# Moving side work between engines in a recurrence-plus-dense kernel: weight remainders to VectorE, weighing to ScalarE, eight full-height turns, and a new order of steps

## The chip, the cores and the metric

One Trainium2 chip, one core. The time is the device time of one execution in microseconds (us); less is better. Engines are named as the profile does: PE is TensorE, DVE is VectorE, ACT is ScalarE, POOL is GpSimd, SP is SyncE.

## The reference

Three layers over x of shape 4 x 768 x 384 (batch, sequence, model), all in fp32. The first is a recurrence for 4 batches and 8 heads of 48 features:

```
for t in range(768):
    y[t]  = r[t] @ (state + outer(u * k[t], v[t]))
    state = w[t][:, None] * state + outer(k[t], v[t])
# token and channel mixing
u2 = x + (relu(x.T @ w_tok1) @ w_tok2).T        # 768 -> 256 -> 768
x  = u2 + relu(u2 @ w_ch1) @ w_ch2              # 384 -> 1536 -> 384
# gated convolution, 5 taps along the sequence
out = (sigmoid(conv(x, conv_w)) * (x @ w_val)) @ w_out
```

## The kernel before

**The recurrence** is worked in super-units of 256 time steps of one batch: s = 0 to 11, three for each batch. Keys k and queries r of two heads lie on 112 partitions (48, 16 of zeros, 48), 1024 columns each. Inside chunks of 64 steps the decays are joined level by level: L1, L2, L4, L8, L16, L32. At level m TensorE multiplies 64 small products (L), VectorE multiplies half of r and k by decays (`carry`, 112x1024), joins the decays of the level four times as long (`join_decays`, a short product) and takes the products into the matrix A (`into_a`, a predicated copy). `carry(m)` of s waits for TensorE's L(m) of s, and TensorE's L(2m) waits for `carry(m)`. Before them stand F (the first level's operands: a copy of odd columns by ScalarE, and even columns times u, called weighing, by GpSimd) and W (the first decays and `carry(1)`, by VectorE). Behind them: T turns k so that time lies on partitions (TensorE, then a ScalarE copy out of PSUM into `kt_sides`), D makes the state products of the chunks (TensorE, ScalarE copies them to `ds`, GpSimd then steps through the states, `states(s)`), A and B give the outputs, and Z splits the result in a high and a low part (ScalarE, then VectorE).

**The dense layers** work on fp32r with each operand split into a high and a low part: three products for one. P and G1 are the first token product, U the second, C1 and C2 the channel products (6 groups for each tile of 256 tokens, 18 matmuls for each group), X, tap, gate, V, M, S, O the gated convolution.

**Weights** come in 20 chunks (w:0 to w:19) through two landing buffers that `gate` and `xf` lend. For each chunk ScalarE writes the high part, and another engine subtracts it to give the low part: VectorE for even chunks, GpSimd for odd ones. The chunk after next may land only when that is done (`w_lo`).

**Order.** Each engine runs its own queue in order. All queues are cut from one list of words: PROLOGUE (batch 0's recurrence, three super-units interleaved, and the first 11 weight chunks), TRIP three times (dense layers of one batch interleaved with the recurrence of the next; n in `L8:n` is the super-unit, 3 being the next batch's first, and `L8:0` the one that the prologue or the trip before began), and TAIL (dense layers of the last batch). A word that an engine has no part in costs it nothing. PSUM for the recurrence is three pairs of banks, in dense stretches two, filled in turn; a stage waits until what it overwrites has been taken out (`emptied`).

Of the kernel before, what the change touches and what calls it, by code (L numbers as in the profile page):

```python
# [5 lines left out]
F32 = mybir.dt.float32  # L6
# [42 lines left out]
def slot(par, p):  # L49
# [5 lines left out]


PROLOGUE = """
    F:0 W:0 L2:0 L1:0 F:1 W:1 L4:0 w:0 L2:1 L8:0 L4:1 F:2 L1:1 w:1 W:2 L16:0 L8:1 L2:2 L1:2 w:2 w:3 L4:2 L16:1
    L32:0 L8:2 w:4 L32:1 T:0 L16:2 D:0 w:5 L32:2 T:1 w:6 D:1 A:0 T:2 B:0 A:1 Z:0 F:3 w:7 w:8 B:1 D:2 Z:1 P:0
    L1:3 A:2 w:9 W:3 L2:3 w:10 B:2 Z:2 P:1 L4:3 P:2 G1.0.0 G1.0.1  # L60
"""
TRIP = """
    L8:0 w:11 U.0.0 w:12 L16:0 w:13 C1.0.0 L32:0 w:14 C1.0.1 T:0 w:15 w:16 C2.0.0 D:0 F:1 C1.0.2 W:1 C2.0.1
    C1.0.3 w:17 C2.0.2 A:0 L1:1 B:0 Z:0 C2.0.3 C1.0.4 L2:1 C1.0.5 L4:1 C2.0.4 w:18 w:19 C2.0.5 X.0.0 L8:1 U.1.0
    L16:1 C1.1.0 L32:1 C2.1.0 tap.0.0 tap.0.1 T:1 C1.1.1 tap.0.2 D:1 C1.1.2 gate.0.0 tap.0.3 V.0.0 A:1 M.0.0 B:1
    C2.1.1 Z:1 tap.0.4 gate.0.1 F:2 S.0.0 C2.1.2 M.0.1 W:2 S.0.1 C1.1.3 C1.1.4 L2:2 C2.1.3 L4:2 O.0.0 L8:2
    C1.1.5 L16:2 L1:2 C2.1.4 L32:2 C2.1.5 X.1.0 U.2.0 T:2 tap.1.0 C1.2.0 D:2 tap.1.1 tap.1.2 C1.2.1 gate.1.0
    tap.1.3 F:3 tap.1.4 C2.2.0 C1.2.2 A:2 V.1.0 W:3 gate.1.1 M.1.0 B:2 C2.2.1 M.1.1 Z:2 C1.2.3 C2.2.2 S.1.0
    S.1.1 O.1.0 L2:3 L1:3 C2.2.3 C1.2.4 C1.2.5 C2.2.4 C2.2.5 X.2.0 tap.2.0 tap.2.1 G1.0.0 tap.2.2 G1.0.1 V.2.0
    tap.2.3 gate.2.0 M.2.0 tap.2.4 gate.2.1 S.2.0 M.2.1 S.2.1 L4:3 O.2.0  # L70
"""
TAIL = """
    U.0.0 C1.0.0 C1.0.1 C2.0.0 C1.0.2 C2.0.1 C1.0.3 C2.0.2 C1.0.4 C2.0.3 C1.0.5 C2.0.4 C2.0.5 X.0.0 U.1.0
# [3 lines left out]
    C2.2.2 O.1.0 C1.2.4 C2.2.3 C1.2.5 C2.2.4 C2.2.5 X.2.0 tap.2.0 N.2.0 V.2.0 tap.2.1 tap.2.2 gate.2.0 tap.2.3  # L77
    M.2.0 tap.2.4 gate.2.1 S.2.0 M.2.1 S.2.1 N.2.1 O.2.0
"""
PAIR_STAGES = tuple(f"L{m}" for m in LEVELS) + ("T", "D", "A")  # L80


# [63 lines left out]
def landing(s):  # L146

    return {0: 2, 1: 0, 2: 3, 3: 1}.get(s, s % 2)
# [58 lines left out]
def build(nc, rk, v, w, u, mask_d, ident_d, tok1_d, tok2_d, ch1_d, ch2_d, val_d, conv_d, outw_d, y_out):  # L207
    ctx = ExitStack()
    with ctx:
# [130 lines left out]
        def emptied(s, name):  # L340

            if name == "T":
                return kt_sb, s + 1
            if name == "D":
                return ds_sb, s + 1
            if name == "A":
                return xl_done, s + 1
            return into_done[landing(s)], INTO[(s, name)] + copies(s, name)
# [62 lines left out]

        @block.gpsimd
        def _(pool):
            def split_weight(n):
                if n % 2 == 1:
                    name, c0, cols, _ = chunks[n]
                    pool.wait_ge(w_hi, n + 1)
                    nc.gpsimd.tensor_tensor(wt[name][:, LO, c0:c0 + cols], stage[1][:, 0:cols],
                                            wt[name][:, HI, c0:c0 + cols].bitcast(F32), ALU.subtract)\
                        .then_inc(w_lo[1], 1)  # L420

            def weigh(s):

                pool.wait_ge(rk_in[landing(s)], 16 * landings(s))
                need(pool, lev_done[1], 4 * tenant(s))
                plain, first = rk_sides[landing(s)][0:RD, 0:1], first_rk[home(s)][0:RD, 0:1]
                steps = [[PH * CH + 1, 2], [QS * CH, PAIRS], [2, SU // 2]]
                scale = bass.AP(ut.tensor, ut.offset, [[ut.ap[0][0], RD], [0, 2], [1, PAIRS], [0, SU // 2]])
                nc.gpsimd.tensor_tensor(bass.AP(first.tensor, first.offset, [list(first.ap[0])] + steps),
                                        bass.AP(plain.tensor, plain.offset, [list(plain.ap[0])] + steps),  # L430
                                        scale, ALU.mult).then_inc(weighed, 1)

            def states(s):

                first = QS * (s % SUPERS)
                need(pool, y_done, 4 * (s - 1))
                pool.wait_ge(decay_done[CH], s + 1)
                pool.wait_ge(ds_sb, s + 1)
                decay = decays(s, CH).rearrange("p (a q) -> p a q", q=QS)
                for q in range(chunks_of(s)):  # L440
                    now, new = st[0:RD, (first + q) % SLOTS], st[0:RD, (first + q + 1) % SLOTS]
                    if first + q == 0:
                        nc.gpsimd.tensor_copy(new, ds[0:RD, q]).then_inc(st_done, 1)
                    else:
                        pool.wait_ge(st_done, states_until(s, q))
                        nc.gpsimd.tensor_tensor(new, now, decay[:, :, q].unsqueeze(2).to_broadcast([RD, PAIRS, D]),  # L446
                                                ALU.mult).then_inc(st_decayed, 1)
                        pool.wait_ge(st_decayed, states_until(s, q) - s // SUPERS)
                        nc.gpsimd.tensor_tensor(new, new, ds[0:RD, q], ALU.add).then_inc(st_done, 1)  # L449

            pool.wait_ge(u_in, 16)
            for kind, n, name in PROGRAM:
                if kind == "weight":
                    split_weight(n)
                elif kind == "att" and name == "F":
                    weigh(n)
                elif kind == "att" and name == "D":
                    states(n)

        @block.scalar  # L460
        def _(act):
# [10 lines left out]
            def first_operands(s):  # L472
# [5 lines left out]
                copy(bass.AP(first.tensor, first.offset, [list(first.ap[0])] + steps),  # L478
                     bass.AP(plain.tensor, plain.offset, [list(plain.ap[0])] + steps)).then_inc(plain_done, 1)

            def att(s, name):
                if name == "F":
                    first_operands(s)
                elif s < SUPERS and name in BY_SCALAR:
                    bank, m = bank_of(s, name), int(name[1:])
                    act.wait_ge(lev_done[m], 4 * (s + 1))
# [7 lines left out]
                                .then_inc(into_done[landing(s)], 1)  # L494
                elif name == "T":
                    bank = bank_of(s, name)
                    act.wait_ge(kt_done, 4 * (s + 1))
                    copy(kt_sides[landing(s)].rearrange("p (w h) d -> p w (h d)", w=2),
                         ps[:, bank:bank + 2, 0:PH // 2 * D]).then_inc(kt_sb, 1)
                elif name == "D":  # L500
                    bank = bank_of(s, name)
                    n = chunks_of(s)
                    act.wait_ge(ds_done, 4 * (s + 1))
                    need(act, st_done, states_until(s, 0))
                    copy(ds[0:RD, 0:n, :, :].rearrange("p q (w a) d -> p w q (a d)", w=2),
                         ps[0:RD, bank:bank + 2, 0:n * 2 * D].rearrange("p w (q e) -> p w q e", q=n))\
                        .then_inc(ds_sb, 1)
                elif name == "Z":
                    bank = bank_of(s, "A")
                    b, i = divmod(s, SUPERS)  # L510
                    act.wait_ge(y_done, 4 * (s + 1))
                    if b:
                        act.wait_ge(mm_done, ring_filled(RING_USE[(b - 1, "U", i, 1)]))
                    copy(xs[:, HI, 2 * i:2 * i + 2, :], ps[:, bank:bank + 2, 0:DM]).then_inc(xh_done, 1)
# [67 lines left out]
        def _(dve):  # L582
# [2 lines left out]

            def split_weight(n):

                if n % 2 == 0:
                    name, c0, cols, _ = chunks[n]
                    dve.wait_ge(w_hi, n + 1)  # L590
                    nc.vector.tensor_tensor(wt[name][:, LO, c0:c0 + cols], stage[0][:, 0:cols],
                                            wt[name][:, HI, c0:c0 + cols].bitcast(F32), ALU.subtract)\
                        .then_inc(w_lo[0], 1)

            def join_decays(s, m):

# [9 lines left out]
            def carry(s, m):  # L606
# [10 lines left out]
                else:  # L617
                    dve.wait_ge(lev_done[m], 4 * (s + 1))
                    dve.wait_ge(decay_done[m], s + 1)
                    if m == 2:  # L620
                        dve.wait_ge(weighed, s + 1)
                mul(both, both, decay).then_inc(next_done[m], 1)

            def into_a(s, name):
# [139 lines left out]
        def _(pe):  # L764
# [28 lines left out]

            def turn_back(s, bank):

                for at0, (p2, q) in enumerate((p2, q) for p2 in range(2) for q in range(QS)):
                    for two in range(2):
                        ph = (2 * two + p2) * QS + q
                        for par in range(2):
                            rows, turn = slice(par * CH, par * CH + D), slot(par, 2 * two)  # L800
                            ins = mm(ps[turn * CH:(turn + 1) * CH, bank + two, at0 * D:(at0 + 1) * D],
                                     k_sides[landing(s)][rows, ph * CH:(ph + 1) * CH], ident[rows, rows], True)
                            if at0 == PH // 2 - 1:
                                ins.then_inc(kt_done, 1)

            def state_products(s, bank):

# [36 lines left out]
            def att(s, name):  # L844
# [3 lines left out]
                        pe.wait_ge(*emptied(*before))  # L848
                if name == "L1":
                    pe.wait_ge(plain_done, s + 1)  # L850
                    pe.wait_ge(weighed, s + 1)
                    scores(s, bank, CH, first_k[home(s)],
                           lambda rows, ph: first_r[home(s)][rows, ph * CH:(ph + 1) * CH], lev_done[1])
                elif name[0] == "L":
# [7 lines left out]
                    pe.wait_ge(next_done[CH // 2], s + 1)  # L862
                    turn_back(s, bank)
                elif name == "D":
                    pe.wait_ge(kt_sb, s + 1)
                    pe.wait_ge(v_in[s % 2], 16 * (s // 2 + 1))
                    state_products(s, bank)
                elif name == "A":
# [196 lines left out]
```

## Time and profile before

| | |
|---|---|
| median of 3 runs | 653.58 us (650.83 to 656.93) |
| the profiled execution | 653.66 us, span 651.9 us |
| busy: PE, PEld, DVE | 605.5, 583.3, 410.1 us |
| busy: ACT, POOL | 185.2, 97.2 us |
| mean granted clock of TensorE | 0.992 |
| chain that ended last | PE 80%, DVE 11%, issue 4%, ACT 2%, POOL 1% |

PE is time in matmuls, PEld in loading their stationary operand, which runs beside PE. The chain is followed back from the last instruction through whatever released each step; "issue" is time for which the profile shows no cause.

### The profile page before, as it was taken

The numbers are of one execution on the slowest core, as the hardware profiler recorded it, in microseconds if no ns is written. First come the engines' busy times: TensorE is split into PE (matmuls) and PEld (weight loads), VectorE is DVE, ScalarE is ACT, GpSimd is POOL, SyncE is SP. The second block draws the span as 40 slices with busy tenths as digits, with TensorE's granted clock in tenths as the row PEclk, the third lists the DMA queues.
The fourth block names the chain that finished last, engine by engine and source line by source line (L and its number), as shares of the span: only waits on it lengthen the run. The fifth ranks groups of instructions, "written<-read, shape, count | busy, mean of one in ns | idle before, by whom it ended". The sixth has DMA issues, their size and how long they took to land.

```text
span 651.9 us, 24065 instructions
## 1 busy us (share of the span) xinstructions
PE 605.5 (93%) x11150; PEld 583.3 (89%) x11150; DVE 410.1 (63%) x618; ACT 185.2 (28%) x323; POOL 97.2 (15%) x110
## 2 busy tenths in 40 slices
PE   3578688999999999999999999999999999999997
PEld 3477587999999999999999999998999989999997
DVE  6996567486678476486678476485676262452616
ACT  2135414224224132213223132213223132221312
POOL 2314812503003000404003000404002000000000
PEclk9999978999999999999999999999999999999999
DMA  9911643410301300300401300300000000000000
GB/s 248 256 29 53 176 132 99 128 34 4 112 27 39 98 1 28 88 25 4 111 28 44 93 1 27 98 17 3 3 27 2 25 7 19 2 1 25 1 25 25
DMA packets 13332, 35.27 MB, mean 54 GB/s; under 512 B 1584, under 2 KB 7984, under 8 KB 11888
## 3 DMA queue, kind: packets, MB, share of 16 engines
q1 hardware_dynamic: 9776, 29.01, 15.9%
q10 hardware_dynamic: 3456, 4.72, 2.0%
q8 instruction: 88, 1.44, 0.9%
q14 instruction: 12, 0.10, 0.1%
HBM read 29.01 MB, written 4.72 MB: 52 GB/s over the span
## 4 chain that ended last, share of the span: by engine, by line
PE 80%; DVE 11%; issue 4%; ACT 2%; DMA 1%; DVEq 1%; POOL 1%; SPq 0%; ACTq 0%; POOLq 0%
PE ps L766 80%; DVE rk L584 2%; DVE wp L584 2%; DVE at L644 1%; DMA w<-in_w_dram 1%; DVE gate L733 1%; DVE rk_next L584 1%; DVEq L708 1%; DVE us L692 1%; ACT x2s L463 1%; DVE x2s L720 1%; DVE xf L709 1%; DVE xf L713 1%; DVE gate L584 0%; DVE x_sum L673 0%
## 5 line engine op out<-in xcount | busy, mean ns | idle before, releaser
L766 PE MATMUL ps<-us,ch 128*128 128x256 f32 x1296 | 167.8, 284 | 2.3 <-DVE us L692 1.7
L766 PE MATMUL ps<-hid,ch 128*128 128x256 f32 x1296 | 165.9, 283 | 0.0
L766 PEld LDWEIGHTS ps<-us,ch 128*128 128x128 f32 x1296 | 158.1, 189 | 5.3 <-DVE us L692 2.9
L766 PEld LDWEIGHTS ps<-hid,ch 128*128 128x128 f32 x1296 | 157.1, 188 | 1.6
L677 DVE SCALAR_TENSOR_TENSOR hid<-ps,hid 128x512 fp32r<-128x512 f32 x72 | 49.7, 691 | 126.9 <-ACT hid L533 126.7
L533 ACT ACTIVATE hid<-ps 128x512 fp32r<-128x512 f32 x72 | 43.0, 598 | 163.0 <-PE ps L766 163.0
L733 DVE SCALAR_TENSOR_TENSOR gate<-xf,cw,gate 128x256 f32<-128x256 f32 x144 | 72.4, 548 | 3.7 <-ACT gate L549 2.7
L766 PE MATMUL ps<-rk 48*64 48x32 f32 (+1 forms) x2240 | 48.4, 244 | 24.8 <-DVE rk L584 19.4
L766 PEld LDWEIGHTS ps<-rk 48*64 48x64 f32 (+1 forms) x2240 | 44.6, 162 | 29.4 <-issue 26.1
L446 POOL TENSOR_TENSOR st<-st,wp 112x192 f32<-112x192 f32 x40 | 23.6, 590 | 194.3 <-ACT ds L463 191.8
L584 DVE TENSOR_TENSOR rk<-rk,wp 112x1024 f32<-112x1024 f32 x35 | 42.9, 1229 | 14.1 <-PE ps L766 14.1
L584 DVE TENSOR_TENSOR rk_next<-rk_next,wp 112x1024 f32<-112x1024 f32 x25 | 33.8, 1351 | 16.9 <-PE ps L766 16.9
L766 PE MATMUL ps<-outw,x2s 128*128 128x384 f32 x216 | 40.3, 339 | 2.0 <-ACT x2s L463 1.8
L766 PE MATMUL ps<-x2s,val 128*128 128x256 f32 x324 | 41.4, 284 | 0.0
L766 PEld LDWEIGHTS ps<-x2s,val 128*128 128x128 f32 x324 | 39.9, 191 | 0.4 <-DVE hid L677 0.2
L766 PEld LDWEIGHTS ps<-outw,x2s 128*128 128x128 f32 x216 | 36.7, 188 | 3.1 <-DVE gate L584 2.2
L644 DVE COPY_PREDICATED at<-masks,ps 128x512 f32<-128x512 uint8 (+1 forms) x36 | 33.7, 936 | 6.8 <-PE ps L766 5.8
L766 PEld LDWEIGHTS ps<-rk_next 48*64 48x64 f32 (+1 forms) x1600 | 24.4, 131 | 9.8 <-issue 7.9
L766 PE MATMUL ps<-rk_next 48*64 48x32 f32 (+1 forms) x1600 | 27.2, 217 | 5.5 <-DVE rk_next L584 5.3
L766 PE MATMUL ps<-tok,h 128*128 128x256 f32 x216 | 31.5, 290 | 0.3 <-DVE h L677 0.2
L644 DVE COPY_PREDICATED at_next<-masks,ps 128x512 f32<-128x512 uint8 (+1 forms) x30 | 27.3, 911 | 4.3 <-PE ps L766 4.0
L449 POOL TENSOR_TENSOR st<-st,ds 112x192 f32<-112x192 f32 x40 | 28.3, 707 | 3.1
(84 smaller groups left out, 630.1 us busy)
## 6 DMA issues: line engine op xcount, KB each, us to landing
rk<-in_rk_dram SPq DMA_DIRECT2D x7, 896.0 KB, 7.2
w<-in_w_dram SPq DMA_DIRECT2D x12, 448.0 KB, 4.2
vs<-in_v_dram SPq DMA_DIRECT2D x12, 384.0 KB, 7.1
out_dram<-gate ACTq DMA_DIRECT2D x24, 192.0 KB, 1.9
rk_next<-in_rk_dram SPq DMA_DIRECT2D x5, 896.0 KB, 6.6
gate<-in_moe_w_ch_dram SPq DMA_DIRECT2D x6, 384.0 KB, 3.3
xf<-in_moe_w_ch_dram SPq DMA_DIRECT2D x6, 384.0 KB, 3.4
gate<-in_moe_w_tok_dram SPq DMA_DIRECT2D x2, 384.0 KB, 9.7
```

Of the source, the lines that this page charges most:

```text
L446: nc.gpsimd.tensor_tensor(new, now, decay[:, :, q].unsqueeze(2).to_broadcast([RD, PAIRS, D]), ALU.mult).then_inc(st_decayed, 1)
L449: nc.gpsimd.tensor_tensor(new, new, ds[0:RD, q], ALU.add).then_inc(st_done, 1)
L463: return nc.scalar.activation(out, in_, ACT.Copy)
L533: nc.scalar.activation(hid[:, HI, g % 2, :], ps[:, RING + use % 2, :], ACT.Relu)\
L584: return nc.vector.tensor_tensor(out, a, b_, ALU.mult)
L644: nc.vector.copy_predicated(out, may.unsqueeze(1).to_broadcast(list(out.shape)), src)\
L677: return nc.vector.scalar_tensor_tensor(out, bank, 0.0, hi.bitcast(F32), ALU.max, ALU.subtract)
L692: nc.vector.tensor_tensor(us[:, LO, dts, :], bank, us[:, HI, dts, :].bitcast(F32), ALU.subtract).then_inc(ring_free[use % 2], 1)
L708: dve.drain()
L709: nc.vector.tensor_tensor(xf[:, :, HALO:], us[:, HI, :, :].bitcast(F32), us[:, LO, :, :].bitcast(F32), ALU.add)
L733: nc.vector.scalar_tensor_tensor(gate3[:, dt, :], xf[:, dt, k:k + TT], cw[:, dt, k:k + 1], gate3[:, dt, :], ALU.mult, ALU.add).then_inc(ta ...
L766: return nc.tensor.matmul(out, lhsT, rhs, start=start, stop=stop, skip_group_check=True, **kw)
```

## The change

Four edits:

- GpSimd makes no low parts of weights any more; VectorE makes all twenty, in its own order.
- Weighing (F) moves from one GpSimd instruction (112x1024) to four ScalarE instructions (112x256 each), behind ScalarE's own copy in F. `weighed` counts to 4 for each super-unit.
- T: 64 small matmuls against a 48x48 identity become eight full-height passes (112 rows, 128 columns of k, identity of 112 columns, transpose mode). ScalarE's single copy of 128x768 out of PSUM becomes four copies of 64x384, which put each quarter to its rows; `kt_sb` counts to 4.
- PROLOGUE and TRIP are in a new order: in the prologue L1:1, L16:1, L32:0, L1:3 and B:2 come earlier and L1:2 and L2:3 later; in the trip C2.0.2 moves behind Z:0, C1.0.0 before w:13, C1.0.4 and C1.0.5 behind one level each, tap.2.3 before G1.0.1. TAIL is unchanged.

```
-    F:0 W:0 L2:0 L1:0 F:1 W:1 L4:0 w:0 L2:1 L8:0 L4:1 F:2 L1:1 w:1 W:2 L16:0 L8:1 L2:2 L1:2 w:2 w:3 L4:2 L16:1
-    L32:0 L8:2 w:4 L32:1 T:0 L16:2 D:0 w:5 L32:2 T:1 w:6 D:1 A:0 T:2 B:0 A:1 Z:0 F:3 w:7 w:8 B:1 D:2 Z:1 P:0
-    L1:3 A:2 w:9 W:3 L2:3 w:10 B:2 Z:2 P:1 L4:3 P:2 G1.0.0 G1.0.1
+    F:0 W:0 L2:0 L1:0 F:1 W:1 L4:0 w:0 F:2 L1:1 L2:1 L8:0 L4:1 w:1 W:2 L16:0 L8:1 L2:2 L16:1 w:2 L32:0 w:3 L4:2
+    L1:2 L8:2 w:4 L32:1 T:0 L16:2 D:0 w:5 L32:2 T:1 w:6 D:1 A:0 T:2 B:0 A:1 w:7 Z:0 F:3 B:1 w:8 D:2 L1:3 Z:1 P:0
+    A:2 w:9 W:3 B:2 Z:2 L2:3 w:10 P:1 L4:3 P:2 G1.0.0 G1.0.1
-    L8:0 w:11 U.0.0 w:12 L16:0 w:13 C1.0.0 L32:0 w:14 C1.0.1 T:0 w:15 w:16 C2.0.0 D:0 F:1 C1.0.2 W:1 C2.0.1
-    C1.0.3 w:17 C2.0.2 A:0 L1:1 B:0 Z:0 C2.0.3 C1.0.4 L2:1 C1.0.5 L4:1 C2.0.4 w:18 w:19 C2.0.5 X.0.0 L8:1 U.1.0
+    L8:0 w:11 U.0.0 w:12 L16:0 C1.0.0 w:13 L32:0 w:14 C1.0.1 T:0 w:15 w:16 C2.0.0 D:0 F:1 C1.0.2 W:1 C2.0.1
+    C1.0.3 w:17 A:0 L1:1 B:0 Z:0 C2.0.2 C2.0.3 L2:1 C1.0.4 L4:1 C1.0.5 C2.0.4 w:18 w:19 C2.0.5 X.0.0 L8:1 U.1.0
-    S.1.1 O.1.0 L2:3 L1:3 C2.2.3 C1.2.4 C1.2.5 C2.2.4 C2.2.5 X.2.0 tap.2.0 tap.2.1 G1.0.0 tap.2.2 G1.0.1 V.2.0
-    tap.2.3 gate.2.0 M.2.0 tap.2.4 gate.2.1 S.2.0 M.2.1 S.2.1 L4:3 O.2.0
+    S.1.1 O.1.0 L2:3 L1:3 C2.2.3 C1.2.4 C1.2.5 C2.2.4 C2.2.5 X.2.0 tap.2.0 tap.2.1 G1.0.0 tap.2.2 tap.2.3 G1.0.1
+    V.2.0 gate.2.0 M.2.0 tap.2.4 gate.2.1 S.2.0 M.2.1 S.2.1 L4:3 O.2.0
...
+TURNS = ((0, 0), (1, 1), (0, 1), (1, 0))
...
-                return kt_sb, s + 1
+                return kt_sb, len(TURNS) * (s + 1)
...
-            def split_weight(n):
-                if n % 2 == 1:
-                    name, c0, cols, _ = chunks[n]
-                    pool.wait_ge(w_hi, n + 1)
-                    nc.gpsimd.tensor_tensor(wt[name][:, LO, c0:c0 + cols], stage[1][:, 0:cols],
-                                            wt[name][:, HI, c0:c0 + cols].bitcast(F32), ALU.subtract)\
-                        .then_inc(w_lo[1], 1)
...
-                nc.gpsimd.tensor_tensor(bass.AP(first.tensor, first.offset, [list(first.ap[0])] + steps),
-                                        bass.AP(plain.tensor, plain.offset, [list(plain.ap[0])] + steps),
-                                        scale, ALU.mult).then_inc(weighed, 1)
...
-                if kind == "weight":
-                    split_weight(n)
-                elif kind == "att" and name == "F":
-                    weigh(n)
-                elif kind == "att" and name == "D":
+                if kind == "att" and name == "D":
...
+            def weigh(s):
+
+
+                for p in range(PAIRS):
+                    at, steps = p * QS * CH, [[PH * CH + 1, 2], [2, SU // 2]]
+                    plain, first = rk_sides[landing(s)][0:RD, at:at + 1], first_rk[home(s)][0:RD, at:at + 1]
+                    nc.scalar.activation(bass.AP(first.tensor, first.offset, [list(first.ap[0])] + steps),
+                                         bass.AP(plain.tensor, plain.offset, [list(plain.ap[0])] + steps),
+                                         ACT.Copy, scale=ut[0:RD, p:p + 1]).then_inc(weighed, 1)
...
                     first_operands(s)
+                    if s == 0:
+                        act.wait_ge(u_in, 16)
+                    weigh(s)
...
-                    act.wait_ge(kt_done, 4 * (s + 1))
-                    copy(kt_sides[landing(s)].rearrange("p (w h) d -> p w (h d)", w=2),
-                         ps[:, bank:bank + 2, 0:PH // 2 * D]).then_inc(kt_sb, 1)
+                    act.wait_ge(kt_done, s + 1)
+                    for row, half in TURNS:
+
+                        to = kt_sides[landing(s)].rearrange("p (w n half) d -> p w n half d", w=2, half=2)
+                        turned = ps[half * CH:(half + 1) * CH, bank, slot(row, 0) * CH:slot(row, 0) * CH + 1]
+                        other = ps[half * CH:(half + 1) * CH, bank + 1, slot(row, 2) * CH:slot(row, 2) * CH + 1]
+                        copy(to[row * CH:(row + 1) * CH, :, :, half, :],
+                             bass.AP(turned.tensor, turned.offset,
+                                     [list(turned.ap[0]), [other.offset - turned.offset, 2], [RD, PH // 4], [1, D]]))\
+                            .then_inc(kt_sb, 1)
...
-                if n % 2 == 0:
-                    name, c0, cols, _ = chunks[n]
-                    dve.wait_ge(w_hi, n + 1)
-                    nc.vector.tensor_tensor(wt[name][:, LO, c0:c0 + cols], stage[0][:, 0:cols],
-                                            wt[name][:, HI, c0:c0 + cols].bitcast(F32), ALU.subtract)\
-                        .then_inc(w_lo[0], 1)
+                name, c0, cols, _ = chunks[n]
+                dve.wait_ge(w_hi, n + 1)
+                nc.vector.tensor_tensor(wt[name][:, LO, c0:c0 + cols], stage[n % 2][:, 0:cols],
+                                        wt[name][:, HI, c0:c0 + cols].bitcast(F32), ALU.subtract)\
+                    .then_inc(w_lo[n % 2], 1)
...
-                        dve.wait_ge(weighed, s + 1)
+                        dve.wait_ge(weighed, PAIRS * (s + 1))
...
-                            ins = mm(ps[turn * CH:(turn + 1) * CH, bank + two, at0 * D:(at0 + 1) * D],
-                                     k_sides[landing(s)][rows, ph * CH:(ph + 1) * CH], ident[rows, rows], True)
-                            if at0 == PH // 2 - 1:
-                                ins.then_inc(kt_done, 1)
+
+                for two in range(2):
+                    for n in range(PH // 4):
+                        first = (two * PH // 4 + n) * 2 * CH
+                        ins = mm(ps[:, bank + two, n * RD:(n + 1) * RD],
+                                 k_sides[landing(s)][0:RD, first:first + 2 * CH], ident[0:RD, 0:RD],
+                                 n == 0, is_transpose=True)
+                ins.then_inc(kt_done, 1)
...
-                    pe.wait_ge(weighed, s + 1)
+                    pe.wait_ge(weighed, PAIRS * (s + 1))
...
-                    pe.wait_ge(kt_sb, s + 1)
+                    pe.wait_ge(kt_sb, len(TURNS) * (s + 1))
```

## Rows read from the trace of the kernel before

**Rows 1.** The page: busy us (share of the span) and instructions of each engine.

```profile
PE 605.5 (93%) x11150; PEld 583.3 (89%) x11150; DVE 410.1 (63%) x618; ACT 185.2 (28%) x323; POOL 97.2 (15%) x110
```

**Rows 2.** Windows: length, busy us of PE, PEld, DVE, ACT, POOL; clock, DMA share, GB/s.

```profile
20.00:30.00 10.00, 5.74 (x196) 5.53 (x200) 10.00 (x10) 2.07 (x2) 5.04 (x2) 1.00 1.02 283
...
83.00:84.00 1.00, 1.00 (x52) 1.00 (x47) 0.00 (x0) 0.00 (x0) 0.00 (x0) 0.50 1.06 350
...
150.00:160.00 10.00, 10.00 (x195) 9.62 (x194) 6.99 (x15) 4.74 (x6) 3.41 (x6) 1.00 0.02 5
```

**Rows 3.** The chain that ended last, in time: start us, us, what.

```profile
63.94 0.82 ACT ds L463
64.88 0.78 POOL st L446
```

**Rows 4.** Timeline of VectorE (DVE), 14 to 103 us: start us, us, instruction.

```profile
14.21 1.99 DVE L584 TENSOR_TENSOR wp<-wp 112x128 f32<-112x128 f32 x1
...
18.72 0.67 DVE L584 TENSOR_TENSOR wp<-w 112x512 f32<-112x512 f32 x1
...
42.25 0.28 DVE L584 TENSOR_TENSOR wp<-wp 112x128 f32<-112x128 f32 x1
...
78.94 2.32 DVE L584 TENSOR_TENSOR wp<-w 112x512 f32<-112x512 f32 x1
...
92.00 1.22 DVE L584 TENSOR_TENSOR rk_next<-rk_next,wp 112x1024 f32<-112x1024 f32 x1 [2.82 <-PE ps L766]
...
102.18 2.85 DVE L584 TENSOR_TENSOR rk_next<-rk_next,wp 112x1024 f32<-112x1024 f32 x1
```

**Rows 5.** Timeline of GpSimd (POOL), same columns.

```profile
13.45 2.60 POOL L429 TENSOR_TENSOR fk<-rk,ut 112x1024 f32<-112x1024 f32 x1 [4.25 <-DMA rk<-in_rk_dram]
...
101.81 2.14 POOL L418 TENSOR_TENSOR ch<-xf,ch 128x768 fp32r<-128x768 f32 x1 [3.99 <-ACT ch L463]
```

**Rows 6.** Groups by form: operation, shapes, count, then busy us and mean ns.

```profile
L463 ACT ACTIVATE gate<-ps 128x384 f32<-128x384 f32 x23 | 11.0, 491 | 47.1 <-PE ps L766 47.1
...
L463 ACT ACTIVATE rk<-ps 128x768 f32<-128x768 f32 x7 | 5.7, 811 | 9.8 <-PE ps L766 9.8
...
L463 ACT ACTIVATE at<-ps 16x256 f32<-16x256 f32 x12 | 4.5, 374 | 18.5 <-PE ps L766 18.3
...
L591 DVE TENSOR_TENSOR tok<-gate,tok 128x768 fp32r<-128x768 f32 x2 | 1.9, 940 | 0.0
```

**Rows 7.** Timeline of TensorE (PE), 79 to 110 us.

```profile
79.08 0.68 PE L766 MATMUL ps<-vs,at 64*64 64x48 f32 x32 [1.48 <-POOL st L449]
...
82.54 1.60 PE L766 MATMUL ps<-rk_next 48*64 48x32 f32 x64 [2.31 <-DVE rk_next L584]
...
87.28 3.52 PE L766 MATMUL ps<-xs,tok 128*128 128x384 f32 x12
...
91.79 2.35 PE L766 MATMUL ps<-xs,tok 128*128 128x384 f32 x12
...
95.41 1.67 PE L766 MATMUL ps<-tok,h 128*128 128x256 f32 x12 [0.20 <-DVE h L677]
96.92 0.60 PE L766 MATMUL ps<-ident,x_sum 128*128 128x128 f32 x4
97.27 0.97 PE L766 MATMUL ps<-tok,h 128*128 128x256 f32 x6
...
105.18 0.75 PE L766 MATMUL ps<-rk_next 48*32 48x32 f32 x64 [2.37 <-DVE rk_next L584]
...
109.16 1.64 PE L766 MATMUL ps<-ident,rk_next 48*64 48x48 f32 x64
```

**Rows 8.** Timeline of TensorE in the second trip, 256 to 261 us.

```profile
256.51 1.15 PE L766 MATMUL ps<-ident,rk 48*64 48x48 f32 x64
257.59 2.38 PE L766 MATMUL ps<-hid,ch 128*128 128x256 f32 x18
259.90 0.94 PE L766 MATMUL ps<-vs,rk 64*48 64x48 f32 x64
```

More of the change, by code:

```diff
@@ L413, in _ @@
         def _(pool):
-            def split_weight(n):
-                if n % 2 == 1:
-                    name, c0, cols, _ = chunks[n]
-                    pool.wait_ge(w_hi, n + 1)
-                    nc.gpsimd.tensor_tensor(wt[name][:, LO, c0:c0 + cols], stage[1][:, 0:cols],
-                                            wt[name][:, HI, c0:c0 + cols].bitcast(F32), ALU.subtract)\
-                        .then_inc(w_lo[1], 1)
[L422 to L428, printed above, removed]
-                nc.gpsimd.tensor_tensor(bass.AP(first.tensor, first.offset, [list(first.ap[0])] + steps),
-                                        bass.AP(plain.tensor, plain.offset, [list(plain.ap[0])] + steps),
-                                        scale, ALU.mult).then_inc(weighed, 1)
             def states(s):
@@ L449, in states @@
                         nc.gpsimd.tensor_tensor(new, new, ds[0:RD, q], ALU.add).then_inc(st_done, 1)
-            pool.wait_ge(u_in, 16)
             for kind, n, name in PROGRAM:
-                if kind == "weight":
-                    split_weight(n)
-                elif kind == "att" and name == "F":
-                    weigh(n)
-                elif kind == "att" and name == "D":
+                if kind == "att" and name == "D":
                     states(n)
@@ L794, in turn_back @@
             def turn_back(s, bank):
[L796 to L800, printed above, removed]
-                            ins = mm(ps[turn * CH:(turn + 1) * CH, bank + two, at0 * D:(at0 + 1) * D],
-                                     k_sides[landing(s)][rows, ph * CH:(ph + 1) * CH], ident[rows, rows], True)
-                            if at0 == PH // 2 - 1:
-                                ins.then_inc(kt_done, 1)
+                for two in range(2):
[5 more added lines that the diff above has]
+                ins.then_inc(kt_done, 1)
             def state_products(s, bank):
```

## The prediction

> **What bounds the kernel now.** I read the page first, then windows of 10 us, then the chain of waits in order of time, then each engine's timeline where TensorE stood idle. The page has TensorE busy for 605.5 of 651.9 us [rows 1], so only some 46 us can be won by closing gaps; the rest needs less work on TensorE. The windows show two regimes. From 110 us on, in the trips, TensorE is busy all through (10.00 of 10 us at 150 us, VectorE 6.99) [rows 2]: only fewer or shorter matmuls help there, and a new wait hurts if it outlasts its cover. In the prologue VectorE is full (10.00 of 10 us at 20 us, TensorE 5.74) [rows 2]; 11 of TensorE's idle us lie before its first matmul, where the change does nothing, and about 26 between 10 and 110 us.
>
> Much of VectorE's time there is not work. A `join_decays` product of 112x128 takes 1.99 us at 14.21 and 0.28 us at 42.25 [rows 4]. At 13.45 GpSimd had begun its 2.60 us weighing, which ends at 16.05, and the VectorE product ends at 16.20 [rows 4, 5]: an instruction of VectorE with both inputs in SBUF stands until GpSimd's is through. This happens four times between 14 and 41 us, each for about 1.65 us, and three times where TensorE waits next: the first decays of super-unit 3 at 78.94 (2.32 us against 0.67 at 18.72), and `carry` before 99 us and at 102.18 (2.85 us against 1.22 at 92.00) [rows 4], the last beside GpSimd's weight chunk at 101.81 [rows 5]. Each of the three costs 1.63 to 1.65 us. The Trainium skill, page "SBUF — State Buffer", rules of the shared port pair, says that whoever starts first holds it for the whole instruction and the other blocks fully; by that rule, the trace agrees, all seven go when GpSimd's two jobs go.
>
> **The change part by part.**
>
> Prologue to 62 us (first stretch). Four stalls of 1.65 us go: -6.6. VectorE takes over w:1 and w:3 there, 0.94 us each [rows 6]: +1.9. A new wait stands at w:2: its high part is now behind ScalarE's copies of L16:1 (four at 0.374 us [rows 6], 1.5 us), and VectorE reaches it after its 1.2 us carry; copies plus high part (0.84 us) make 2.4 us, so VectorE waits 1.0. Queued behind it are carries on which TensorE depends: +1.0. The chain is then no longer VectorE's alone, since TensorE's stages take 1.6 to 1.9 us each here (1.14 from 75 us on, at the same granted 1.00), and the order has L16:1 and L32:0 ahead, so that L32:1 and T:0 follow at once. T:0 and T:1 are cheaper on TensorE and dearer on ScalarE (below), which nearly cancels. I take -4.5 for this stretch, between -6.6 (nothing new waits) and -2 (TensorE's stages take over at once).
>
> Weighing on ScalarE. No row shows it from SBUF at 256 columns; the nearest is the 16x256 copy, 0.374 us [rows 6], so about 1.6 us for four, and at most 2.0 if each takes the 0.491 of 384 columns. It comes after the 1.17 us copy in F, so `weighed` is complete some 1 us later than GpSimd made it. For s = 0 to 2 the first user (L1 on TensorE, `carry(2)` on VectorE) starts over 2 us after that. In the trips, ScalarE is busy 28% [rows 1]. Behind F:1 stands the relu of C1.0.2, which will be about 1.5 us late, but its user C2.0.2 now comes behind C2.0.1, C1.0.3, A:0, L1:1 and B:0, some 9 us of TensorE. Price 0, at worst 12 x 1.6 = 19 us if nothing covered it.
>
> From 62 to 79 us everything hangs on latencies: D:1, ScalarE's `ds` copy at 63.94, GpSimd's states at 64.88 [rows 3], A:1, B:1, D:2, the states again, A:2 at 79.08 [rows 7]. GpSimd's own weight chunks did not sit in front of the states, so nothing is won or lost: 0. F:3 now lies before D:2's copy on ScalarE; T:2, w:7, Z:0, F:3 and w:8 make 2.0 + 0.8 + 0.8 + 2.8 + 0.8 = 7.2 us after T:2, and D:2 ends about 7.5 us after it: just covered.
>
> From 79 to 95 us (second stretch). A:2 starts at 79.08; then TensorE waits 2.31 us for the carry of super-unit 3, runs L2:3 at 82.54 and only then B:2, drops to the lower clock (granted 0.50, 1.2 of 2.4 GHz) at 83 us [rows 2, 7], and gets P:1 done in 3.52 us where P:2, 12 matmuls of the same shape, takes 2.35 at full clock [rows 7]. U starts at 95.41 [rows 7]. In the new order B:2 follows A:2 at once, and the carry is earlier by the 1.65 us stall and because L1:3 moved ahead of P:0. From 79.08 on: A:2 and B:2 2.2, L2:3 1.1, P:1 2.35, L4:3 1.1, P:2 2.35, L8:3 1.1, 0.6 for h's low part: 10.8 us, so U at 89.9 in old time: -5.5. If the clock falls all the same, -3.5.
>
> From 95 to 110 us (third stretch). The old U to the old T:3 took 13.75 us (95.41 to 109.16), with 2.37 us of waiting for the stalled carry before L32:3 and half clock again (T:3 1.64 us against 1.15) [rows 7, 8]. VectorE loses two stalls of 1.63 and gains w:11 and w:13, 1.9 us. The critical carry before L32:3 is then 1.4 us sooner against U, and C1.0.1 and T:3 run at full clock (C1.0.1 2.3 in place of 3.3): -2.2, and -1 if the clock falls.
>
> The turn. In a trip the 64 matmuls hold TensorE from 256.51 to 257.59, 1.08 us [rows 8]. The new passes are of the kind of U's four transposes of x_sum, which hold it from 96.92 to 97.27 [rows 7], 0.0875 us each; eight make 0.70. Nine turns lie in the trips: the first at half clock now (-0.9), eight at -0.38: -3.9 in all. Taken at their full 0.272 us each, with no overlap, they would be 2.2 us and the nine turns +9; the back-to-back row decides. The skill's page "TensorEngine Tiling (Array Packing)", restrictions, says that column tiling rules out the fp32 transpose mode, so the old form could not have it; that fits the 0.0875, and no row shows a small matmul in that mode.
>
> The four copies behind T have 384 columns each, 0.491 us [rows 6], so 2.0 us where one took 0.811 [rows 6]: +1.15 us before D may start. Cover: between T and D stands one group of 18 matmuls (257.59 to 259.90, 2.31 us) [rows 8], and ScalarE needs 0.2 + 2.0. It is hidden by a hair in the trips. Where ScalarE is late with a relu, it shows. I book 0.2 for each of nine: +2.
>
> In the trips VectorE's new order of low parts adds a wait for each odd chunk, which GpSimd used to take. Behind w:15 and w:16 stand the relu remainders of C1, and C2's last terms. A landing buffer cycles in 3.4 (landing) + 0.84 + 0.94 = 5.2 us, and the words leave 5 to 6 us between chunks of one buffer: 0, at worst 2.
>
> Sum: -4.5 - 5.5 - 2.2 - 3.9 + 2.0 = -14.1 on 653.66, the profiled execution, which stands at the median of 653.58: **639.6 us, I say 640**.
>
> **The rivals.** (1) The prologue passes from VectorE to other links. TensorE's slow early stages, ScalarE's longer queue (T:0, L16:2, D:0, w:5, L32:2, T:1 make 8.5 us in a row) and the clock, which falls in the same two places, leave -2 - 3.5 - 1 of the first three stretches; with -3.9 and +2 that is -8.4: 645. For it: many of VectorE's neighbours are nearly as late. Against: all three critical stalls were seen to release TensorE directly. (2) It does not do what it says: the seven stalls come not from GpSimd's work but from something else VectorE does, and only the turn and the order pay. Then 1.9 x 2 is added, B:2's move gives -3 and the turn -2: about 652. Against it stands that each stalled instruction ends within 0.15 us of GpSimd's. (3) Slower: ScalarE becomes the path in the trips. The deciding point is whether a copy of 64x384 ends within (2.31 - 0.2) / 4 = 0.53 us. If writing to the other half of the rows makes it 0.811, as for 768 columns, T to D takes 3.4 us against 2.31 of cover, 1.1 us for each of twelve, and each such gap is of the size after which the clock fell at 83 us and may cost another 1.1 as at T:3 and C1.0.1. That is +13 to +26, and with -12 from the rest: 655 to 668, say 660. (4) The clock falls by the turns themselves. The six transposes of U at 96.92 to 98.45 ran at granted 1.00 and nothing fell in the next 8 us. The skill's page "TensorE: Matmul & The Clock Gate", part on PE-mode transpose, says that a transpose does not count as busy for the gate; by that rule each T would pull toward half clock. As a mechanism here, a fall for 3 us after each of nine turns costs 1.5 us apiece, +13 on the forecast: 653. The rows on x_sum speak against it.
>
> **How the numbers follow.** Forecast 0.62 (634 to 645), rival 1 0.22 (643 to 649), rival 2 0.05, rival 3 0.06, rival 4 0.05. The range of 8 in 10 reaches from 633 (no new waits, -6.6 in the first stretch, early stages shorter) to 649. Within about 1% a measurement here can't tell a change from none: faster by that, under 647.1, has the forecast and most of rival 1, 0.83; within it the rest of rival 1, and rivals 2 and 4, 0.12; slower, rival 3, 0.05.
>
> **What would show it.** VectorE: no product of 112x128 or less above 0.5 us in the prologue, carries at 1.22 throughout, ten more low parts at 0.94; busy total about the same as before. GpSimd down to some 55 us, ScalarE up to about 218. L2:3 after B:2 with no wait over 1 us, clock 1.00 throughout, U near 85 and T:3 near 97 us. T in a trip 0.7 us, D behind it with no gap. The forecast fails if a 64x384 copy takes over 0.53 us, if eight passes take over 1.1 us, or if VectorE is found waiting for high parts in front of a carry.

## The result and the profile after

The changed kernel takes 642.63 us (median of 4 runs, 641.92 to 644.56) against 652.75 before (650.83 to 656.93): a ratio of 0.9839, 95% interval 0.9808 to 0.9869. The forecast was 640 in a range of 633 to 649. On another chip, beside the last experiments, it was 642.40 against 654.79, 0.9813 (0.9774 to 0.9852).

The page of the profiled execution (644.56 us, span 642.5), its busy line to be held against [rows 1]:

```profile
PE 603.5 (94%) x10478; PEld 581.8 (91%) x10478; DVE 398.5 (62%) x628; ACT 217.5 (34%) x407; POOL 51.7 (8%) x88
...
q8 instruction: 82, 1.34, 0.9%
```

The work went where it was sent: GpSimd 97.2 to 51.7 us, ScalarE 185.2 to 217.5 (forecast 218). VectorE took ten more low parts and is still 11.6 us less busy, since its instructions no longer stand while GpSimd does those two jobs. TensorE's busy time fell by only 2.0 us; the other 7.4 of the 9.4 us that the span lost are idle time.

VectorE's timeline, the answers to [rows 4]:

```profile
13.92 0.28 DVE L582 TENSOR_TENSOR wp<-wp 112x128 f32<-112x128 f32 x1
...
77.39 1.08 DVE L582 TENSOR_TENSOR wp<-w 112x512 f32<-112x512 f32 x1
...
101.86 1.21 DVE L582 TENSOR_TENSOR rk_next<-rk_next,wp 112x1024 f32<-112x1024 f32 x1
```

All seven stalls by GpSimd's two jobs are gone. Small ones beside GpSimd's states are left: the first decays at 77.39 take 1.08 us against 0.68 undisturbed, and a `carry` at 58.05 takes 1.61 against 1.22. TensorE's timeline, the answers to [rows 7], with what stands in the prologue now:

```profile
19.89 1.22 PE L763 MATMUL ps<-fk 48*64 48x64 f32 x33 [2.70 <-issue]
...
26.86 3.75 PE L763 MATMUL ps<-rk 48*64 48x32 f32 x127 [3.34 <-issue]
...
32.49 3.63 PE L763 MATMUL ps<-rk 48*64 48x32 f32 x127 [1.88 <-issue]
...
78.07 0.68 PE L763 MATMUL ps<-vs,at 64*64 64x48 f32 x32 [1.42 <-POOL st L432]
...
81.14 0.77 PE L763 MATMUL ps<-vs,at 64*64 64x48 f32 x18 [1.35 <-issue]
...
84.48 3.47 PE L763 MATMUL ps<-xs,tok 128*128 128x384 f32 x12
...
92.55 1.67 PE L763 MATMUL ps<-tok,h 128*128 128x256 f32 x12 [0.20 <-DVE h L674]
...
103.22 0.96 PE L763 MATMUL ps<-ident,rk_next 112*128 112x112 f32 x8 [0.22 <-DVE rk_next L582]
103.94 2.38 PE L763 MATMUL ps<-hid,ch 128*128 128x256 f32 x18
```

Read as a list of dates against before: T:0 starts 1.3 us sooner (49.88 for 51.19), A:2 1.0 (78.07 for 79.08), U 2.9 (92.55 for 95.41), T:3 5.9 (103.22 for 109.16), the end 9.4. So 5.9 us come before the trips are under way and 3.5 in them. In the prologue the place of the VectorE waits is taken by a kind that names nobody ("issue") and lies in the middle of a stage: 2.70 us behind the first 222 matmuls, then 3.34 and 1.88 us, each behind 127 more. GpSimd's states are held up by VectorE:

```profile
57.39 1.18 POOL L432 TENSOR_TENSOR st<-st,ds 112x192 f32<-112x192 f32 x1
58.65 1.38 POOL L429 TENSOR_TENSOR st<-st,wp 112x192 f32<-112x192 f32 x1
60.11 0.59 POOL L432 TENSOR_TENSOR st<-st,ds 112x192 f32<-112x192 f32 x1
```

An addition of 0.59 us takes 1.18 while VectorE makes a low part at 57.00, and the product behind it 1.38 against 0.51 while VectorE carries at 58.05. The blocking is mutual. It is not new in kind: in the kernel before, such an addition had taken 1.45 us at 59.98, beside a `carry` of VectorE. New are the low parts that VectorE makes beside the states. The last addition before A:2 takes 1.34 us, beside the low part of w:9 at 76.53:

```profile
76.58 1.34 POOL L432 TENSOR_TENSOR st<-st,ds 112x192 f32<-112x192 f32 x1
```

### The profile page after: what moved, and what is told of

It reads as the page before. It is cut to its first block, busy times and chain, and to the rows that moved or that the text cites. A ratio compares the mean times of both kernels' runs of the same rounds, so it can differ in the third digit from the quotient of the medians.

```text
span 642.5 us, 22783 instructions
## 1 busy us (share of the span) xinstructions
PE 603.5 (94%) x10478; PEld 581.8 (91%) x10478; DVE 398.5 (62%) x628; ACT 217.5 (34%) x407; POOL 51.7 (8%) x88
## 3 DMA queue, kind: packets, MB, share of 16 engines
q8 instruction: 82, 1.34, 0.9%
## 4 chain that ended last, share of the span: by engine, by line
PE 82%; DVE 6%; issue 4%; ACT 4%; POOL 2%; DMA 1%; DVEq 0%; SPq 0%; ACTq 0%; POOLq 0%
PE ps L763 82%; DVE gate L730 3%; POOL st L432 1%; DMA w<-in_w_dram 1%; POOL st L429 1%; ACT gate L547 1%; DVE rk L582 1%; DVE hid L674 1%; DVE rk_next L582 1%; DVE us L689 1%; ACT fk L465 1%; DVE ch L588 0%; ACT x2s L441 0%; ACT hid L531 0%; ACT fk L441 0%
## 5 line engine op out<-in xcount | busy, mean ns | idle before, releaser
L730 DVE SCALAR_TENSOR_TENSOR gate<-xf,cw,gate 128x256 f32<-128x256 f32 x144 | 69.7, 530 | 3.7 <-ACT gate L547 2.7
L582 DVE TENSOR_TENSOR rk_next<-rk_next,wp 112x1024 f32<-112x1024 f32 x25 | 30.5, 1221 | 17.3 <-PE ps L763 17.3
L441 ACT ACTIVATE x2s<-xf 128x512 fp32r<-128x512 f32 (+1 forms) x24 | 11.3, 517 | 55.8 <-DVE xf L710 55.8
```

The lines of the kernel that those rows point to most:

```text
L441: return nc.scalar.activation(out, in_, ACT.Copy)
L582: return nc.vector.tensor_tensor(out, a, b_, ALU.mult)
L730: nc.vector.scalar_tensor_tensor(gate3[:, dt, :], xf[:, dt, k:k + TT], cw[:, dt, k:k + 1], gate3[:, dt, :], ALU.mult, ALU.add).then_inc(ta ...
```

## The experiments

Each time stands beside that of the kernel before on the same chip, and ratios are to that. The series ran on different chips, so their times are compared by the ratios. Dates and waits are those of one execution of each kernel. The first four undo one part of the change each, or two; the second four test causes; the last four the turn by itself and the gains together.

**Both GpSimd jobs back.** (The edit is shown shortened.)

```
 for kind, n, name in PROGRAM:          # GpSimd
+    if kind == "weight":
+        split_weight(n)                # odd chunks
+    elif kind == "att" and name == "F":
+        weigh(n)
     elif kind == "att" and name == "D":
         states(n)
```

> The changed kernel with both GpSimd jobs back on GpSimd (odd low parts and weighing); order and turn stay new. If VectorE's blocking by GpSimd was what the change removed, the product at 14 us takes 1.9 us again, TensorE reaches T:0 at 52 us or later in place of 49.9, and the time is 646 to 650 us. If the new order and the turn pay for everything, it is 641 to 643 us.

651.44 us against 654.94: 0.9951 (0.9924 to 0.9978), span 649.5. The product at 14 us is at 1.99 us again:

```profile
14.48 1.99 DVE L593 TENSOR_TENSOR wp<-wp 112x128 f32<-112x128 f32 x1
```

So GpSimd's reads are what VectorE stood for: rival 2 falls. But TensorE reaches T:0 at 50.97 us, not at 52 or later as I had expected, and T:3 at 104.60 against 103.22: most of the loss isn't in the prologue. From T:3 to the last T the run takes 379.3 us, the changed kernel 373.6. TensorE's waits from 110 to 520 us, in total, times, longest:

```profile
PE ps L775 <- POOL fk L431: 4.3, 3, 2.2
PE ps L775 <- DVE hid L686: 1.5, 2, 0.8
```

Once in each trip L1:1 waits for GpSimd's weighing, which lies behind its states. The old order had C2.0.2 in between. After the longest of these waits (2.23 us, up to 118.49) the granted clock is at its lower level from 120.1 to 123.5 us, and the 36 matmuls there take 5.72 us, where 36 of the same shape take 4.49 in the changed kernel. The waits and this fall make 5.5 of the 5.7 us.

**The old order.** PROLOGUE and TRIP as before, all else changed.

> The changed kernel with PROLOGUE and TRIP in the old order. My theory: B:2 stands behind L2:3 again, the old order also leaves F:3 in the same place of the trip, so the loss is 2 to 4 us, 645 to 647 us. Rival, that the order is the whole gain: 650 us or more. Rival, that the order does nothing since TensorE waits for its own instructions: 642 to 643 us.

643.15 us against 654.94: 0.9821 (0.9783 to 0.9858). Span 642.9 against 642.5; T:3 starts at 104.07 in place of 103.22. With the jobs moved and the new turn the order is worth nothing that can be measured; the interval leaves room for some 3 us either way. I had expected 2 to 4 us. The dates show two things that cancel: from A:2 to U the old order takes 16.5 us against 14.5, but it reaches A:2 at 76.86, 1.2 us sooner.

**The old turn.** `turn_back` and ScalarE's copy as before, all else changed.

> The changed kernel with the old turn: 64 small matmuls and one copy by ScalarE. By the rows, a turn in a trip holds TensorE 1.08 us against 0.72, nine of them make 3.2 us, less about 1 us that the shorter ScalarE copy gives back: 644 to 646 us. Rival, the turn's saving is eaten by its four copies: 642 to 643 us. Rival, fewer instructions are what counts: 648 us.

647.98 us against 654.94: 0.9896 (0.9858 to 0.9935). The time is the one that I had given for the last rival, 648, that fewer instructions are what counts. But this chip ran the kernel before 2.2 us slower than the first; by the ratio the run is 3.7 to 5.4 us above the changed kernel's two series, which is above the 1.4 to 3.4 that I expected and reaches the rival's. The run doesn't decide between them. Its profiled execution happened to keep the clock at 1.00 throughout and had a span of 642.8, so dates from its start can't be used; from T:3 to the last T it takes 376.1 us against 373.6. These 2.5 us are all that the trace places.

**Weighing alone back on GpSimd.**

> The changed kernel with weighing alone back on GpSimd. If blocking in the prologue counts: three weighings of 1.9 us at 13, 21 and 69 us block VectorE again, and the time is 644 to 646 us. If ScalarE's load in the trips counts more (in each trip the relu behind F:3 is late and TensorE waits 0.8 us for it), the time is 640 to 642 us.

648.22 us against 654.94: 0.9903 (0.9868 to 0.9938). Slower than I gave even the pessimistic case. Again the trips hold the largest part (377.2 us from T:3 to the last T, against 373.6), and again by waits for `fk`, 3.9 us in three. Taking the load off ScalarE did not take away the wait of 0.8 us in V.1.0 that I had put down to it. TensorE stands there 0.79 us, now because VectorE's taps are held while GpSimd weighs at 197.61: eight take 6.71 us, where they take 5.07 in the changed kernel.

```profile
193.27 6.71 DVE L731 SCALAR_TENSOR_TENSOR gate<-xf,cw,gate 128x256 f32<-128x256 f32 x8
```

**The jobs alone**, on the kernel before.

> The kernel before with only the two GpSimd jobs moved; order and turn old. With jobs back the changed kernel took 651.4 us, with the old order 643.2. If the jobs alone are the change, this takes 645 to 648 us, which is the old order's time plus the turn's 3 us. If the jobs pay only in the new order, where L1:1 follows the states sooner and waited for GpSimd's weighing (4.3 us in three trips), it takes 649 us or more.

649.36 us against 653.10: 0.9944 (0.9915 to 0.9973). That is 3.7 us less, where the first stretch and the two later stalls had been counted at some 6, and it falls in the second case of the expectation (649 or more).

**F:3 earlier in the trip.**

```
-C1.2.1 gate.1.0 tap.1.3 F:3 tap.1.4
+C1.2.1 F:3 gate.1.0 tap.1.3 tap.1.4
```

> The changed kernel with F:3 moved in the trip from behind gate.1.0 to ahead of it, into a stretch of 3.2 us in which ScalarE waits for VectorE's taps; only ScalarE takes part in F. If the late relu of C1.2.2 is the new wait (TensorE 0.8 us in V.1.0, once in a trip), those three waits go and the time falls by 2 to 2.5 us against the changed kernel, to about 640 us. If another link is as late, it moves by less than 0.5 us.

639.69 us against 653.10: 0.9781 (0.9745 to 0.9817). In the changed kernel TensorE stood in V.1.0:

```profile
200.64 1.34 PE L763 MATMUL ps<-x2s,val 128*128 128x256 f32 x9 [0.82 <-DVE hid L674]
```

This happens in two trips, 0.82 and 0.74 us; in the third there is no F:3, and no such wait. VectorE was late with C1.2.2's remainder because ScalarE's relu had to queue behind F:3, 2.8 us long. That is one half of it. In the run with the old turn, where F:3 is as long, the wait is shorter:

```profile
198.89 1.34 PE L756 MATMUL ps<-x2s,val 128*128 128x256 f32 x9 [0.35 <-DVE hid L667]
```

There ScalarE copies once behind T:2 (0.82 us) and not four times (2.01), and reaches C1.2.0's relu, which starts the taps, 0.57 us sooner behind T:2. So about 0.35 us of each wait belong to weighing and the rest comes with the new turn. With F:3 ahead of gate.1.0, ScalarE fills a stretch in which it waited:

```profile
190.28 1.16 ACT L441 ACTIVATE fk<-rk 112x1024 f32<-112x1024 f32 x1
191.31 1.79 ACT L465 ACTIVATE fk<-rk,ut 112x256 f32<-112x256 f32 x4
193.61 0.63 ACT L551 ACTIVATE gate<-gate 128x512 f32<-128x512 f32 x1 [0.51 <-DVE gate L730]
```

No wait of TensorE for `hid` is left, and from T:3 to the last T it takes 371.5 us in place of 373.6. That is 2.1 us less in the trips (1.4 against the second series), at the lower end of what I expected, for two waits and not the three that I had counted.

**Early loads later.** (Shown shortened; `cw` are the taps.)

```
-load_v(0)
 load_weight(1)
-load_v(1); load cw; load_rk(3)
...
     load_weight(n + 2)
+    if n == 1:
+        load_v(0); load_v(1); load cw; load_rk(3)
```

> The changed kernel with the first two loads of v, the taps and super-unit 3's r and k issued about 13 to 20 us later. TensorE now stands 2.7, 3.3 and 1.9 us between 17 and 33 us in the middle of a stage, each time after about 128 matmuls, with the DMA engines full. If it waits there for its own instructions behind the data transfers, the stand of 3.3 us at 24 us shrinks to about 1 us and T:0 starts 1 to 2 us sooner. Rival, a semaphore that the profile doesn't name or a fixed cost of a fetch: the stands keep their lengths, whatever the DMA engines do.

639.09 us against 653.10: 0.9778 (0.9741 to 0.9815).

```profile
19.82 1.22 PE L764 MATMUL ps<-fk 48*64 48x64 f32 x33 [2.96 <-issue]
...
24.33 6.69 PE L764 MATMUL ps<-rk 48*64 48x32 f32 x227 [0.87 <-issue]
```

The first stand, before which the same transfers run as ever, keeps its length (2.96). The second falls from 3.34 to 0.87, the third (1.88) is gone, and T:0 starts at 46.65, 3.2 us sooner than in the changed kernel. That date is of one execution: in the two runs further down that have this edit too, the second stand is 1.69 and 1.43 us, but T:0 starts at 48.05 and at 50.94, the latter behind a stand of 3.49 us at 41 us. With the loads early T:0 starts between 49.5 and 50.3 in four executions. The second stand is shorter in all three, then; what is left of that at T:0 differs. The stands follow the load on the DMA engines: I take it that TensorE waits for something that comes by DMA and isn't data, since no semaphore is named and the stage is half done. Between two stands lie 127 or 128 matmuls with as many weight loads. The instruction queue's row on the page of the kernel before (queue: packets, MB, share):

```profile
q8 instruction: 88, 1.44, 0.9%
```

That is 16.4 KB a packet; the changed kernel has 82 packets, 1.34 MB, and 1282 instructions fewer. All of this fits a fetch of some 256 instructions at a time; no run shows the fetch itself.

**Super-unit 4's load later.** `load_rk(4)` at B:2 in place of B:1.

> The changed kernel with super-unit 4's r and k (896 KB) loaded behind B:2 in place of B:1. TensorE stands 1.35 us in the middle of B:2 at 79.8 us, and the clock falls to 0.50 at 80.5 us for some 6 us. If that stand is a fetch behind this load, it falls to under 0.8 us; if the clock's fall hangs on it, the clock stays at 1.00, and P:1 takes 2.35 us in place of 3.47: 2 us less in all. Rival: the fall hangs on the wait for the states before A:2 (1.42 us) and stays.

643.54 us against 653.10: 0.9844 (0.9799 to 0.9889). The stand in B:2 is gone, the clock falls all the same (columns as in [rows 2]):

```profile
79.00:80.00 1.00, 1.00 (x52) 1.00 (x55) 0.54 (x2) 0.00 (x0) 0.00 (x0) 0.69 0.72 259
80.00:81.00 1.00, 1.00 (x49) 1.00 (x46) 0.00 (x0) 0.27 (x1) 0.00 (x0) 0.50 0.75 147
```

The rival's sign holds: the fall to the lower level (1.2 GHz) doesn't hang on that stand. TensorE had been idle for 1.42 us up to 77.67 before it; that this wait is the cause isn't shown.

**The changed kernel again.**

> The changed kernel again, on the chip of the three runs beside it. The comparisons so far were each made against the kernel before on another chip. It should take 641.5 to 644 us; the clock should fall once between 57 and 87 us or not at all, and the span follow it by about 2 us.

642.40 us against 654.79. Its profiled execution had a span of 638.8; T:3 starts at 100.21 in place of 103.22. That is how much one execution differs from another, and it is made between A:2 and U. Both executions reach A:2 at 78.0 us. In the first, the slowest of its four, the clock is at the lower level from 80.1 to 86.9 us, in B:2, L2:3 and P:1, and U follows A:2 by 14.5 us. In this one, the fastest of its five, it was low from 72.2 to 75.6 us, ahead of a wait for the states (0.93 us before A:2) that takes up what it cost, and U follows by 11.5. Of these 3 us, 0.7 are a shorter stand in B:2.

**The turn alone**, on the kernel before.

> The kernel before with the new turn alone. With jobs and order new, taking the new turn away cost 5.4 us by the medians, where the rows of nine turns in the trips make 3.2. If the rest comes from the prologue (56 fewer matmuls in each turn, so fewer stands of TensorE for instructions), this takes 4 to 6 us less than the kernel before, 648 to 650. If only the trips' turns count, 2 to 3.5 us less; if ScalarE's four copies cost more where GpSimd still blocks VectorE, no less at all.

648.93 us against 654.79: 0.9911 (0.9876 to 0.9946), -5.9. From T:3 to the last T, 373.6 us against 376.7: 3.1 us. That is as much as eight turns of 0.38, but it doesn't come in equal parts: T:3 alone, at half clock before, gives 0.87, and behind each T:2 TensorE now waits 0.40 us for `us` and in two trips 0.73 for `hid`. The other 2.6 us of the profile come before T:3. TensorE's unexplained waits from 8 to 110 us, before and here:

```profile
PE ps L766 <- issue: 7.8, 8, 1.4
```

```profile
PE ps L774 <- issue: 3.4, 4, 2.2
```

The stand of 1.4 us between L32:2's matmuls at 57 us is one that went. That looks like the reason for the 2.6 us, but the dates say otherwise. By A:2 nothing is won (79.78 us against 79.08), since the waits for GpSimd's states grew from 2.8 to 6.1 us:

```profile
79.78 1.11 PE L774 MATMUL ps<-vs,at 64*64 64x48 f32 x32 [4.11 <-POOL st L450]
```

All of it comes behind A:2. The wait of 2.31 us for the `carry` before L2:3 is covered by the long wait before A:2, and there is no second fall of the clock before T:3.

**The two helpful edits together.**

> The changed kernel with both edits that helped: F:3 ahead of gate.1.0 in the trips, and the first loads of v, the taps and super-unit 3's r and k issued later. They touch different stretches, so their 2.9 and 3.5 us should add: 636 to 638 us. If both only bought the same luck with the clock in the prologue, 639 us.

637.47 us against 654.79: 0.9746 (0.9702 to 0.9789), 4.9 below the changed kernel on the same chip.

**All three.**

> The same with super-unit 4's load behind B:2 as well. It took away the stand in B:2 (1.35 us) but not the clock's fall. If stands for instructions count where nothing else waits, it gives up to another 1 us, 635 to 637; if the clock's fall sets the end of that stretch, the same time as the run beside it.

636.82 us against 654.79: 0.9734 (0.9694 to 0.9774). The third edit adds nothing that can be told apart.

## Why the prediction was right, point by point

| kernel | jobs | order | turn | ratio to before |
|---|---|---|---|---|
| turn alone | | | new | 0.9911 |
| jobs back | | new | new | 0.9951 |
| jobs alone | new | | | 0.9944 |
| old turn | new | new | | 0.9896 |
| old order | new | | new | 0.9821 |
| changed, two series | new | new | new | 0.9839, 0.9813 |

Each ratio is good to about 0.003 or 0.004, some 2 us, so two of the table differ for certain only by 3 us and more. Where dates from T:3 on are compared, they are of one execution each, and within the trips those repeat where the clock holds: 373.6 us in the first series of the changed kernel, 372.9 in the second.

The total was 2.6 us too optimistic, and 2.4 under rival 1's 645, so it doesn't choose between the two; the parts do. Up to T:3 the forecast had -12.2 us and rival 1 -6.5; the two executions of the changed kernel show -5.9 and -8.9. From T:3 on the forecast had -1.9, and they show -3.5 and -4.2. The prologue paid less and the trips more than I said. That these misses partly cancel is luck. The signs that I had named for the prologue didn't come: U near 85 and T:3 near 97 us were to be seen, 92.55 and 103.22 were (89.54 and 100.21 in the second series), and the clock fell once.

**VectorE's stalls.** The mechanism was right: the seven stalls by GpSimd's two jobs are gone, and the first is back (1.99 us) when GpSimd gets its reads back. The Trainium skill, page "SBUF — State Buffer", on the shared port pair, states the blocking for both sides; I used one. The trace has the other too, GpSimd's 1.38 us in place of 0.51.

**First stretch.** Forecast -4.5, measured -1.3 at T:0 and -2.1 at D:1, where the stretch ends: the step mis-sized. Its own three terms (-6.6, +1.9, +1.0) made only -3.7; the other 0.8 had no term. VectorE was freed by 6.6 us, but TensorE could not use it, as it stood 8.9 us between 17 and 37 us in those unnamed stands (instructions, as I take it), a link that I had seen as "issue" in the chain and not priced. That is rival 1 in kind, with another cause: not the pace of the stages, nor ScalarE's queue. Moving loads out of that stretch shortened the second stand in all three runs that did it, and gave 3.2 us at T:0 in one execution.

**62 to 79 us.** Forecast 0, measured +1.1. I held that nothing sat in front of the states. VectorE's new low parts did, through the shared reads: states(0) ended late, and D:1's `ds` copy waited for it at 62.65, 0.8 us of it; and the addition at 76.58, which A:2 waits for, took 0.75 us more than undisturbed.

**Second and third stretch.** -5.5 and -2.2 by my sum, -1.9 and -3.1 by the dates. B:2 did move, but TensorE stood 1.35 us in it, and the clock fell at 80.1 as it had at 83, so P:1 took 3.47 us. For that case I had said -3.5. In the second series the clock holds there, and the stretch pays -4.8. The order was credited with all of this; undoing it costs nothing that the times show, as A:2 then comes sooner. In the third stretch there was no second fall, as forecast.

**The turn.** 0.70 us forecast, 0.72 measured (103.22 to 103.94). Its value from T:3 to the last T came out at 3.1 us on the kernel before and 2.5 in the changed one. By the times the turn is worth 5.9 and 3.7 to 5.4 us; where the rest lies isn't shown, and that it comes from fewer instructions to be brought isn't either. In the changed kernel each T:2 gave its gain back: C1.2.0 waits 0.36 to 0.4 us for VectorE's `us`, which the longer turn had covered.

**ScalarE's copies and weighing.** Four copies take 2.01 us (0.50 each, under the 0.53 that would have decided for rival 3), and D follows with no gap in the trips. Weighing takes 1.76, forecast 1.6. I priced F:1 and found it covered, rightly; I did not look at F:3, behind which C1.2.2's relu stands. The wait in V.1.0 comes to 1.6 us in two trips, some 0.7 of it from weighing, which I had priced at 0, and the rest with the turn. With the three waits for `us` (1.2 us) the turn's side costs come to about the +2 that I had booked, in other places than before D.

**Rivals.** 1: right in kind for the first stretch. 2: excluded by the jobs-back run. 3: excluded by the 0.50 us. Its working also misread the rows: a gap of 1.1 us is not of the size after which the clock fell at 83 us, which was 2.31. 4: no turn in the trips was followed by a fall of the granted clock; the rule on transposes of the Trainium skill's page "TensorE: Matmul & The Clock Gate", part on PE-mode transpose, shows no effect here (eight take 0.72 us at granted 1.00, and the clock stays there).

What stays open: what makes the clock fall once in some executions and not in others, where the rest of the turn's gain lies, and what TensorE stands for in the prologue. The jobs are worth 3.7 us alone and 7.3 to 9.0, by the two ratios, under the new order and turn. 4.3 us of the latter are the wait for weighing that the new order exposes, and 1.2 the fall of the clock behind it in the one execution that was traced.

## What to carry to other kernels

When an engine is relieved, ask what the bound engine waits for next, and don't leave out waits that name nobody. Here stands in the middle of a stage, about every 127 small matmuls, grew with the load on the DMA engines, and it paid to issue loads that weren't urgent later. An order and the placement of work belong together: with the jobs on GpSimd the new order made TensorE wait 4.3 us in three trips, and without them it cost nothing. Of a step that moves to another engine, look at every place where it is called, not the first. Before a gain is put down to waits that went, compare the dates behind them: with the turn alone the unnamed waits fell by 4.4 us, and by A:2 nothing had been won.

## What the runs showed of the hardware

- Blocking between VectorE and GpSimd goes both ways: a VectorE product with two SBUF inputs of 0.28 us took 1.99 beside GpSimd's weighing, and a GpSimd product of 0.51 us took 1.38 beside VectorE's. It reaches into the trips: eight taps took 6.71 us beside weighing and 5.07 without it.
- TensorE stands about every 127 matmuls of the small kind, 0.3 to 3.9 us; one of 3.34 to 3.90 us became 0.87 to 1.69 in three runs in which 1.66 MB (896 KB and twice 384 KB) were loaded later.
- Eight fp32 transposes of 112x128 take 0.72 us in a row at granted 1.00; 64 matmuls on quarter tiles for the same data take 1.08.
- Early in the kernel eight turns take 1.68 us (49.88 to 51.56) and a stage of 64 small matmuls 1.7, at a granted clock that is listed as 1.00; after 74 us the same take 0.72 and 1.07. In the second series the faster pace begins at 65 us already. The clock column doesn't tell these apart.
- Where the clock falls counts. In two executions of the changed kernel, 6.8 us at the lower level behind A:2 came with 3 us more from A:2 to U, while 3.4 us at it ahead of A:2, where TensorE then waited for the states, left the date of A:2 at 78.0 us.
